# Splitting the odd heads' q and k on GpSimd, and moving a weight block forward at the start of an attention and two-layer-MLP kernel

## The reference

```python
# q, k, v: (2, 8, 768, 64); centroids: (8, 16, 64)
q_assign = argmax(normed(q) @ normed(centroids).T)     # likewise k_assign
mask = q_assign[..., :, None] == k_assign[..., None, :]
scores = where(mask, 64 ** -0.5 * q @ k.T, -1e9)
x = softmax(scores) @ v            # (2, 8, 768, 64), heads joined: (1536, 512)
x = ((x @ w1) * (x @ w2)) @ w3 @ w_out        # widths 1024, 1024, 512
h = x @ w_in                                   # width 2048
out = (maximum(h, 0) + alpha * minimum(h, 0)) @ w_out2   # (1536, 512)
```

## Time and profile before

| | us |
|---|---|
| median of 3 runs | 750.02 |
| lowest, highest | 749.32, 750.09 |
| the profiled execution's own time | 750.02 |
| its span, from first to last instruction | 748.2 |
| TensorE matmul busy | 738.7 (99%) |
| weight loads busy | 639.5 (85%) |
| DVE, ACT, POOL busy | 414.1 (55%), 312.7 (42%), 179.6 (24%) |

### The profile page before, as it was taken

The page is one execution under the profiler, slowest core; times in us unless marked ns, Lnnn a source line. Parts: engine busy times, 40 slices in busy tenths (PEclk is TensorE's granted clock), DMA queues, the critical chain, the costliest instruction groups (busy, mean ns, idle before and its releaser), DMA issues.

```text
span 748.2 us, 10631 instructions
## 1 busy us (share of the span) xinstructions
PE 738.7 (99%) x3778; PEld 639.5 (85%) x3778; DVE 414.1 (55%) x632; ACT 312.7 (42%) x623; POOL 179.6 (24%) x211
## 2 busy tenths in 40 slices
PE   6999999999999999999999999999999999999998
PEld 5888999999999998888888888888888888888886
DVE  4435999999999994731311433475433334343332
ACT  5335988988988884421311332432012111121111
POOL 2141556866865894500000000000000000000000
PEclk9999999999999999999999999999999999999999
DMA  9645476666566333300000032230001000010001
GB/s 293 178 120 133 96 155 151 140 158 145 141 160 147 77 94 83 106 28 1 1 0 1 7 106 62 79 115 27 0 1 57 0 1 1 0 57 1 0 1 56
DMA packets 64858, 55.72 MB, mean 74 GB/s; under 512 B 31520, under 2 KB 53040, under 8 KB 64816
## 3 DMA queue, kind: packets, MB, share of 16 engines
q1 hardware_dynamic: 64816, 55.16, 28.3%
HBM read 31.50 MB, written 3.19 MB: 46 GB/s over the span
## 4 chain that ended last, share of the span: by engine, by line
PE 98%; ACT 1%; POOL 1%; DVE 0%; issue 0%; POOLq 0%
PE slot L621 63%; PE acc L621 24%; PE slot L685 9%; PE acc L634 1%; PE slot L733 1%; ACT xh L934 0%; POOL cwin L464 0%; DVE xl L1152 0%; ACT xh L927 0%; POOL oh L465 0%; DVE abx L1272 0%; DVE ab L1268 0%; ACT abx L1044 0%; ACT asb L1030 0%; ACT ost L1097 0%
## 5 line engine op out<-in xcount | busy, mean ns | idle before, releaser
L621 PE MATMUL slot<-xh,w 128*128 128x512 f32 x768 | 248.0, 389 | 0.0
L621 PEld LDWEIGHTS slot<-xh,w 128*128 128x128 f32 x768 | 144.1, 188 | 30.0
L621 PE MATMUL slot<-xl,w 128*128 128x512 f32 x384 | 149.5, 389 | 0.0
L1090 ACT CAST gh<-gf 128x512 fp32r<-128x512 f32 x48 | 29.9, 623 | 203.2 <-PE acc L621 186.0
L1195 DVE TENSOR_TENSOR pl<-slot,ph 128x384 fp32r<-128x384 f32 x192 | 97.5, 549 | 8.5 <-ACT ph L962 8.2
L1189 DVE TENSOR_REDUCE nm<-slot 128x1 f32<-128x768 f32 x96 | 91.2, 950 | 15.2 <-PE slot L621 13.9
L962 ACT CAST ph<-slot 128x384 fp32r<-128x384 f32 x192 | 83.7, 488 | 33.4 <-PE slot L685 32.6
L954 ACT ACTIVATE pf<-slot,nm 128x768 f32<-128x768 f32 x96 | 88.1, 918 | 6.0 <-DVE nm L1189 5.7
L621 PEld LDWEIGHTS slot<-xl,w 128*128 128x128 f32 x384 | 72.1, 188 | 14.7
L1318 DVE TENSOR_TENSOR gl<-gf,gh 128x512 fp32r<-128x512 f32 x48 | 33.2, 692 | 89.9 <-ACT gh L1090 89.9
L621 PE MATMUL slot<-k,q 96*128 96x384 f32 (+1 forms) x384 | 83.0, 337 | 0.0
(11 more groups left out here) (118 smaller groups left out, 1011.9 us busy)
## 6 DMA issues: line engine op xcount, KB each, us to landing
stage<-in_moe_w SPq DMA_DIRECT2D x16, 256.0 KB, 3.4
stage<-in_moe_w_in SPq DMA_DIRECT2D x16, 256.0 KB, 2.9
stage<-in_moe_w_out SPq DMA_DIRECT2D x16, 256.0 KB, 3.1
stage<-in_moe_w SPq DMA_DIRECT2D x6, 512.0 KB, 4.9
qk<-in_q SPq DMA_DIRECT2D x16, 192.0 KB, 3.8
qk<-in_k SPq DMA_DIRECT2D x16, 192.0 KB, 4.0
vn<-in_v SPq DMA_DIRECT2D x16, 192.0 KB, 3.6
q<-k SPq DMA_DIRECT2D x16, 192.0 KB, 2.8
```

The source lines that it names most:

```text
L621: return nc.tensor.matmul(o, a, b, start=start, stop=stop)
L1090: copy(gh[j % 2][:, :], gf[j % 2][:, :]).then_inc(gh_done, 1)
```

## The change

It does four things.

- **Odd heads' operands.** From head 3 on, ScalarE writes the scaled odd head's half into a new float32 buffer `raw`, and that alone frees the PSUM bank. POOL then makes `q1` and `k1` from `raw` (`operands`), at the head of steps m = 0 and 1. The DVE operation is left out for those heads. The cluster scores and SP's `stack_first` wait for POOL's `split_done`; so does ScalarE before it writes `raw` anew.
- **POOL's order.** `x_hi` and `x_lo` come five steps later (`X_LATER`): at m = 2 and 3 instead of 9 and 10, but for the very last pair. The even heads' `split_v` comes at m = 11 instead of 0. The windows of the next turn still come at the step with m = 11 ahead of it, now after `split_v`.
- **The loop's edge.** LEAD is 16: it lies between m = 3 and m = 4.
- **The front.** Block 1 of w3 is loaded after piece 1 of w_out instead of after piece 3, turned ahead of chunks 4 and 5, and cast and subtracted ahead of piece 3.

`ctab` and `cwin` shrink by parts that weren't read, and DVE counts `hi_done` by even halves.

```diff
@@ -40,3 +40,3 @@
 LT, LW, LX = 4, 5, 6
-LEAD = 2 * T6 - 1
+LEAD = 16
 NPF, NPH = T6, 3
@@ -48,2 +48,3 @@
 FILLS = 6
+X_LATER = 5
 
@@ -130,4 +131,5 @@
         v12 = [sb(f"v12_{i}", [P, T6, P], F32R, attn) for i in range(2)]
-        ctab = sb("ctab", [P, H, 96], F32R, attn)
-        cwin = [sb(f"cwin{j}", [P, 384], F32R, attn) for j in range(HB)]
+        ctab = sb("ctab", [P, H, 64], F32R, attn)
+        cwin = [sb(f"cwin{j}", [P, 256], F32R, attn) for j in range(HB)]
+        raw = sb("raw", [P, 2, HS], F32, attn)
         ct = sb("ct", [P, S], F32, attn)
...
@@ -274,2 +277,6 @@
 
+        def even_halves(it, j, half, first):
+
+            return 2 * j + half + 1 if first and j < 2 else 2 * pair(it, j) + half + 3
+
         def lo_rows(j):
@@ -307,3 +314,6 @@
                 h = j % HB
-                sp.wait_ge(prep_free, fill_of(it, "turned", j, 1) + 1)
+                if j % 2 and j > 1:
+                    sp.wait_ge(split_done, 2 * pair(it, j))
+                else:
+                    sp.wait_ge(prep_free, fill_of(it, "turned", j, 1) + 1)
                 sp.dma_start(q2[h][0:D, :].bitcast(F32), k1[h][0:D, :].bitcast(F32)).then_inc(stacked1[h], 16)
@@ -385,5 +395,6 @@
             sp.dma_start(al16, alpha.rearrange("(j p) -> j p", p=P)).then_inc(ld_al, 16)
-            for i in range(1, NWO):
-                load_wo(i)
+            load_wo(1)
             load_w3(1, 1)
+            for i in range(2, NWO):
+                load_wo(i)
             for f in (2, 3):
...
@@ -520,2 +531,13 @@
 
+            def operands(it, j, half):
+
+                cols, n = slice(half * HS, (half + 1) * HS), 2 * pair(it, j) + half - 1
+                pool.wait_ge(prep_free, fill_of(it, "turned", j, half) + 1)
+                nc.gpsimd.tensor_tensor(q1[j % HB][:, cols], raw[:, half, :],
+                                        zero[:, 0:1].to_broadcast([P, HS]), ALU.add).then_inc(raw_done, 1)
+                pool.wait_ge(raw_done, n)
+                nc.gpsimd.tensor_tensor(k1[j % HB][:, cols], raw[:, half, :],
+                                        q1[j % HB][:, cols].bitcast(F32), ALU.subtract).then_inc(split_done, 1)
+                pool.wait_ge(split_done, n)
+
             def add_epsilon(it, j):
@@ -561,7 +583,11 @@
                 out_head, u = finished(c)
-                for kind, h, _ in prepared(it, c, last):
+                for kind, h, half in prepared(it, c, last):
+                    if kind == "turned" and h % 2:
+                        operands(it, h, half)
                     if kind in ("pick1", "pick2"):
                         picks(it, h, int(kind[4]))
-                if t == 0 and c > 0 and (not last or j < HB):
+                if c % 12 == 6 and (not last or j < HB):
                     split_v(it, j)
+                if c % 12 == 11 and (not last or j + 1 < HB):
+                    split_v(it, j + 1)
                 summed = inverted_now(c, last, 1)
@@ -573,10 +599,12 @@
                     normalise(it, out_head, 1)
-                if u == 3 and out_head % 2:
-                    x_hi(it, out_head)
-                if c == LEAD and not last:
-                    pool.wait_ge(prep_full, FILLS * (2 * it + 2))
-                    for h in range(HB, 2 * HB):
+                if last and out_head == HB - 1 and u >= 3:
+                    x_hi(it, out_head) if u == 3 else x_lo(it, out_head) if u == 4 else None
+                done, v = finished(c - X_LATER)
+                if v in (3, 4) and done % 2 and not (last and done == HB - 1):
+                    x_hi(it, done) if v == 3 else x_lo(it, done)
+                if c % TILES == 11 and not last and (c < TILES or not isinstance(it, int)):
+                    h0 = c // TILES * HB + HB
+                    pool.wait_ge(prep_full, FILLS * (2 * it + h0 // 2))
+                    for h in range(h0, h0 + HB):
                         window(it, h)
-                if u == 4 and out_head % 2:
-                    x_lo(it, out_head)
 
@@ -644,2 +672,4 @@
                 pe.wait_ge(cwin_done, head(it, j + 2))
+                if not first:
+                    pe.wait_ge(split_done, 2 * pair(it, j) + half - 1)
                 for e in range(2):
@@ -773,7 +803,6 @@
             product_wc(0, (2, 3))
-            pe.wait_ge(piece_lo, 3)
-            product_wc(0, (4, 5))
             turn_w3(1, 1)
-            pe.wait_ge(piece_lo, NWO)
-            product_wc(0, (6, 7))
+            for i in range(2, NWO):
+                pe.wait_ge(piece_lo, i + 1)
+                product_wc(0, (2 * i, 2 * i + 1))
             turn_w3(2, 0)
@@ -945,2 +974,7 @@
                 act.wait_ge(prep_full, f + 1)
+                if j % 2 and not first:
+                    if not (isinstance(it, int) and it == 0 and j == 3):
+                        act.wait_ge(split_done, 2 * pair(it, j) + half - 3)
+                    nc.scalar.mul(raw[:, half, :], acc[:, 0, 0:HS], scl[:, 0:1]).then_inc(prep_free, 1)
+                    return
                 nc.scalar.mul(q1[j % HB][:, half * HS:(half + 1) * HS], acc[:, half if first else 0, 0:HS], scl[:, 0:1]
@@ -990,4 +1024,4 @@
             wo_hi(2)
-            wo_hi(3)
             w3_hi_part(1, 1)
+            wo_hi(3)
             w3_hi_part(2, 0)
@@ -1158,3 +1192,3 @@
                 cols = slice(half * HS, (half + 1) * HS)
-                dve.wait_ge(hi_done, 2 * head(it, j) + half + 1)
+                dve.wait_ge(hi_done, even_halves(it, j, half, first))
                 nc.vector.scalar_tensor_tensor(out=k1[j % HB][:, cols], in0=acc[:, half if first else 0, 0:HS],
@@ -1210,3 +1244,4 @@
                     if kind == "turned":
-                        operands_lo(it, j, half)
+                        if j % 2 == 0:
+                            operands_lo(it, j, half)
                     elif kind == "cluster":
@@ -1224,4 +1259,4 @@
             wo_lo(2)
-            wo_lo(3)
             w3_lo_part(1, 1)
+            wo_lo(3)
             centroid_table()
```

More of the change, by code:

```diff
@@ L214, in build @@
         prep_full, prep_free, hi_done = sem("prep_full"), sem("prep_free"), sem("hi_done")
+        raw_done, split_done = sem("raw_done"), sem("split_done")
         cwin_done, v_hi_done, v_done = sem("cwin_done"), sem("v_hi_done"), sem("v_done")
@@ L385, in _ @@
             sp.dma_start(al16, alpha.rearrange("(j p) -> j p", p=P)).then_inc(ld_al, 16)
-            for i in range(1, NWO):
+            load_wo(1)
+            load_w3(1, 1)
+            for i in range(2, NWO):
                 load_wo(i)
-            load_w3(1, 1)
             for f in (2, 3):
@@ L476, in window @@
                 h = HB * ((it + j // HB) % 2) + j % HB
-                nc.gpsimd.tensor_tensor(cwin[j % HB][:, 64:128], ctab[:, h, 0:64].bitcast(F32),
+                nc.gpsimd.tensor_tensor(cwin[j % HB][:, 64:128], ctab[:, h, :].bitcast(F32),
                                         zero[:, 0:1].to_broadcast([P, 64]), ALU.add).then_inc(cwin_done, 1)
@@ L990, in _ @@
             wo_hi(2)
+            w3_hi_part(1, 1)
             wo_hi(3)
-            w3_hi_part(1, 1)
             w3_hi_part(2, 0)
@@ L1224, in _ @@
             wo_lo(2)
+            w3_lo_part(1, 1)
             wo_lo(3)
-            w3_lo_part(1, 1)
             centroid_table()
```

## The result

The changed kernel takes 753.85 us (median of 6 runs, 753.15 to 754.72) against 750.03 us (749.32 to 750.41, 6 runs) of the kernel before: a ratio of 1.0052, with a 95% interval of 1.0039 to 1.0065. It is slower by 3.8 us, half a per cent. Its profiled execution took 753.43 us with a span of 751.6, against 750.02 and 748.2 before, so 3.4 us of the difference can be looked for in the traces: 2.2 lie in the front and 1.2 in attention. The ratios given here leave out executions in the slow state; there were two, of 922 and 923 us, one of e12 and one of the kernel before beside it.

The account below looks back on a forecast made before the run. The prediction took TensorE to set the pace, with DVE nearly full but waiting for it. 750.0 + 1.9 (windows at turn boundaries) + 1.9 (front) = 753.8 us, range 750.8 to 756.5.

Parts of the forecast that it names:

- part 1: Attention, positions 0 and 1: taking the odd heads' split off DVE gains 0, bounds 0 and 2.9 us.
- Part 2: Attention: the split on POOL costs 0 in ordinary pairs, about 0.95 us at each of two turn boundaries, +1.9 us.
- the cluster product: Turn boundary, attention: with four windows ahead of POOL's half 0, this product starts 0.4 us late.
- The pick: Turn boundary, POOL: the first pick ends late, so DVE's next maxima and TensorE behind them wait 0.4 to 0.75 us.
- the loop's edge: Between positions 3 and 4: the loop's jump back delays POOL's first pick, which starts at 156.4 to 156.75.
- Part 3: Front: TensorE waits for the last w_out piece, and the next product starts at 20.5, not 18.62: +1.9 us.
- Part 4: The rest: more unrolled steps, smaller table and windows, earlier even heads' v split, all off the path: 0.
- The first: Rival, attention: DVE sets the pace, so less work on it shortens the stage: 743.4 us, 10%.
- The second: Rival: the pieces cancel, part of the 2.9 us comes back and windows cost nothing: 749.0 to 751.5 us, 12%.
- The third: Rival: only the front costs, POOL being fast enough at the windows: 751.9 us, 12%.
- The fourth: Rival, attention: POOL is late in every pair, five more pairs paying 0.4 us: 755.8 us, 7%.
- The fifth: Rival, front: the hole of 2.3 us takes TensorE back to its lower clock, 3 us more: 756.8 us, 7%.

Follow-up runs that it names:

- e12: e6's kernel with POOL splitting even heads, one-hot transpose at position 9, masks earlier on SP, e3's order; its edit for the last pair met no step: 749.37 us.
- e2: The kernel before with only the changed front's four edits put in: 752.37 us against 749.5, ratio 1.0038.
- e1: The changed kernel with the four edits of the front undone, attention as changed: 750.38 us against 749.5, ratio 1.0014.
- e4: The kernel before with DVE's subtraction for odd heads cut from 384 to 8 columns from head 5 on: 749.69 us against 749.5, ratio 1.0004.
- e6: e1's kernel with the next turn's four windows moved into POOL's waits for DVE, at positions 4 and 6: 749.82 us against 749.55, ratio 1.0005.
- e5: The kernel before with DVE's one-hot transpose at position 8 cut from 768 to 32 columns: 748.36 us against 749.5, ratio 0.9982.
- e8: The kernel before with the changed front's loads and TensorE order, ScalarE's and DVE's order as before: 749.69 us against 749.55, ratio 0.9999.
- e3: The kernel before with only TensorE's new order in the front, loads, ScalarE and DVE as before: 749.14 us against 749.55, ratio 0.9992.

## Why the prediction was right

The forecast was 753.8 us and 753.85 came, with the two mechanisms that it named. That it came within 0.1 us is luck: in the profiled executions the front cost 2.2 us and the attention part 1.2, 3.4 together, where 1.9 and 1.9 stood, and the medians differ by 3.8. By the medians and ratios of e2 and e1 it is 2.85 and 1.05; there too one term is above 1.9 and the other below, and the two errors nearly cancel. The forecast's own bounds have a slip: its parts' lower bounds add up to 750.0 + 0 + 1.6 = 751.6, not 752.3; nothing hangs on it.

**What bounds the kernel, and part 1 (DVE's relief, 0).** Right. e4 took the work away with nothing in return and the time stayed; e6 has it on POOL at no cost and it stayed too. The reading that decided it was DVE's idle 0.32 us ahead of a maximum at position 4, and the changed kernel's 0.49 us ahead of the maxima of positions 1 and 2 are the same thing, larger. By the rule of the Trainium skill, page Perfetto Trace Analysis, section Identifying the Most-Contended Engine, applied to busy shares from 160 to 180 us, DVE was the engine to relieve; the traces agree for one of its operations and not for the other that was tried: 0 us for the subtractions of e4 (0.39 us each), 1.35 us for the transpose of e5. One reading was half wrong: the 2.9 us of waits for `pl` were all put behind the transpose of position 8, and only 1.45 us lie there. e5 takes just these away.

**Part 2 (windows, +1.9).** The mechanism was right, the size 0.7 us too large in the profiled executions (1.2; by e1's ratio 1.05, between 0.4 and 1.7). Step by step: the cluster product was to be 0.4 us late and was 0.24, by which its step grew 0.25 (152.12, where the kernel before with its 2.19 us of offset would have stood at 151.88). The pick was to cost 0.4 to 0.75 and cost 0.62 (2.67 less 2.05): 0.87 for the first boundary against 0.95. The second gave 0.17 and 0.28, 0.45 in all, and here a step failed: the forecast counted the loop's edge at both boundaries. At the second, POOL's pause ahead of the first pick is 0.23 us instead of 0.55; by the program the loop has been left by then and the code goes on unrolled. e1 has the same pauses and, at position 6, 2.67 and 2.31 us. No run moves the edge alone; e6, which has the 0.55 us too, loses nothing to it once the windows are out of the way. This is the row, POOL in the changed kernel:

```profile
215.30 1.03 POOL L517 TENSOR_TENSOR c<-ct 128x384 f32<-128x384 f32 x1 [0.23 <-POOL xl L576]
```

Some 0.1 us is won back at other steps. Ordinary pairs cost nothing, as said: between the boundaries the offset doesn't grow.

**Part 3 (the front, +1.9).** Right in every link that was tested. In e2 the numbers are the forecast's own: the hole ends at 18.20 (forecast 18.2), block 1 starts at 20.48 (20.5). In the changed kernel's execution both are 0.36 us later: the turn began at 13.83 instead of 13.69, and took 0.99 us to the next matmul, where 0.79 was put. e8 confirms the cause, the place of the turned block's cast and subtraction ahead of the last piece's. By the ratio the front costs 2.85 us, and its interval (1.8 to 3.9) holds the forecast at its lower end; whether it is more than 1.9 is open.

**Part 4 (the rest, 0).** Nothing of it shows: with the windows moved as well, e6 is at 1.0005.

**The rivals.** The first (DVE sets the pace, 743.4) falls with e4. The second (pieces cancel) needed part of the 2.9 us back and windows that cost nothing; the steps of position 10 stayed at 2.60 to 2.69 us, the waits for `pl` grew to 4.1, and the windows cost. The third (only the front) falls with e1, whose interval excludes 1. The fourth (POOL late in every pair) didn't come: four steps are long, two at each boundary. The fifth, the lower clock after the hole, didn't either: from 18.56 us matmuls of 512 columns follow each other every 0.23 us, and the granted clock reads 1.00, the 2.4 GHz level, from 8 to 22 us.

## What to carry to other kernels

An engine that is full but waits for the bottleneck once in a round has nothing to give: look for the single step at which the bottleneck waits for it, and take work from there, since a microsecond anywhere else turns into idle time. When an item is pulled forward on one engine, check the order that this forces on the queues behind it: an early turn on TensorE was free, and putting its followers ahead of a piece that was already loaded cost all of it; one DMA behind another's wait cost 11 us. Where a burst that comes once in some rounds (here four windows) meets a fuller queue, put it into that engine's waits for others.

## What the runs showed of the hardware

**The rate at which TensorE starts.** In the first microseconds matmuls of 512 columns follow each other every 0.43 us and later every 0.23, while the granted clock reads 1.00 in both. The change came near 13.69 us in the kernel before, in the changed kernel during the turn, by 14.82, and in e8 near 11.41:

```profile
10.94 0.64 PE L622 MATMUL slot<-xh 128*128 128x512 f32 x1
11.41 0.39 PE L622 MATMUL slot<-xl,xh 128*128 128x512 f32 x1
```

So the length of the front differs by more than a microsecond between executions of the same TensorE instructions: block 1 starts at 17.00 us in e8 and at 18.29 in e3 (e8's profiled execution took 748.41 us, its median is 749.69). A term of the front that is read from one pair of profiles can carry an error of that size. What sets the moment isn't shown.

**This hole didn't bring the slow rate back.** The 2.1 us without work, in the changed kernel and in e2, were followed by matmuls of 512 columns every 0.23 us.

**The price of a loop's edge on POOL.** The pause between `xl` and the first pick is 0.55 us where the loop jumps back in between, 0.17 us inside the loop (ahead of 129.07 and 185.93 us) and 0.23 just behind it. e1 and e6 show the same three values.
